# The second layer's unrolled blocks become a counted loop on four engines

## The reference

```python
# attention: q, k, v are (8 batches, 8 heads, 576 positions, 64)
k_p, v_p = means of k, v over groups of 8 positions        # 72 keys per head
attn = softmax(q @ k_p.T / sqrt(64)) @ v_p
x = attn, laid out as (4608 tokens, 512 features)

h = x @ w_in1                                              # 512 -> 2048
g = where(h >= 1, h, where(h <= -1, 0, (h + 1)**2 / 4))
x2 = g @ w_out1                                            # 2048 -> 512

h = x2 @ w_in2                                             # 512 -> 2048
g = h - tanh(h)
y = g @ w_out2                                             # 2048 -> 512
```

## Time and profile before

| | |
|---|---|
| median of 3 runs | 1790.83 us (1788.91 to 1792.78) |
| the profiled execution | 1790.83 us, its span 1788.9 us |
| TensorE busy | 1737.6 us of the span, 97% |
| VectorE, ScalarE busy | 876.1 us, 543.5 us |
| instructions | 24545 |
| granted TensorE clock, mean | 0.994 |

### The profile page before, as it was taken

How to read it: one execution, slowest core, us unless ns; L and a number is a source line. 1 busy time by engine, 2 the same in 40 slices (tenths; PEclk the granted TensorE clock), 3 DMA queues, 4 the chain that set the end, 5 groups by cost and what they waited for, 6 DMA issues and landing times.

```text
span 1788.9 us, 24545 instructions
## 1 busy us (share of the span) xinstructions
PE 1737.6 (97%) x10480; PEld 1575.3 (88%) x10480; DVE 876.1 (49%) x1745; ACT 543.5 (30%) x1141; POOL 160.5 (9%) x136
## 2 busy tenths in 40 slices
PE   4999999999999999999999999999999999999998
PEld 4999999999999999999999888888888888888887
DVE  6585675766856757668544222222222222222222
ACT  3533333333333333333335222222222222222221
POOL 4700011001100110011006100000000000000000
PEclk8999999999999999999999999999999999999999
DMA  5411012001110020111014101010101010101000
GB/s 170 149 60 64 20 34 77 26 26 66 39 64 26 27 77 26 57 34 39 14 65 138 60 0 48 0 48 0 48 0 48 1 47 1 47 1 47 1 24 24
DMA packets 47628, 78.12 MB, mean 44 GB/s; under 512 B 3488, under 2 KB 19872, under 8 KB 47520
## 3 DMA queue, kind: packets, MB, share of 16 engines
q1 hardware_dynamic: 47520, 76.56, 13.2%
HBM read 57.67 MB, written 18.87 MB: 43 GB/s over the span
## 4 chain that ended last, share of the span: by engine, by line
PE 88%; DVE 8%; ACT 2%; DMA 1%; issue 1%; POOL 0%; SPq 0%; DVEq 0%
PE acc_ps L499 42%; PE h_ps L489 30%; PE att_ps L489 6%; PE score_ps L489 6%; PE score_ps L514 2%; DVE v_sum L860 1%; PE score_ps L534 1%; DVE bent L818 1%; DVE g_lo L811 1%; PE att_ps L526 1%; DVE v_tail L882 1%; DVE h_ps L824 1%; DVE prob L896 1%; DVE row_sum L903 1%; DVE row_max L888 1%; ACT prob L698 1%
## 5 line engine op out<-in xcount | busy, mean ns | idle before, releaser
L499 PE MATMUL acc_ps<-g_hi,wout_hi 128*128 128x288 f32 (+1 forms) x1600 | 540.7, 338 | 5.8 <-ACT prob L698 5.8
L499 PE MATMUL acc_ps<-g_hi,wout_lo 128*128 128x288 f32 (+1 forms) x1600 | 529.4, 331 | 0.0
L499 PE MATMUL acc_ps<-g_lo,wout_hi 128*128 128x288 f32 (+1 forms) x1600 | 529.2, 331 | 0.0
L489 PE MATMUL h_ps<-x_hi,win_hi 128*128 128x288 f32 (+1 forms) x1312 | 423.9, 323 | 17.1 <-DVE g_lo L811 12.9
L489 PE MATMUL h_ps<-x_hi,win_lo 128*128 128x288 f32 (+1 forms) x1312 | 416.9, 318 | 0.0
L489 PE MATMUL h_ps<-x_lo,win_hi 128*128 128x288 f32 (+1 forms) x1312 | 414.1, 316 | 0.0
L499 PEld LDWEIGHTS acc_ps<-g_hi,wout_hi 128*128 128x128 f32 x1600 | 302.7, 189 | 34.7 <-ACT prob L698 9.3
L499 PEld LDWEIGHTS acc_ps<-g_lo,wout_hi 128*128 128x128 f32 x1600 | 303.4, 190 | 25.4
L499 PEld LDWEIGHTS acc_ps<-g_hi,wout_lo 128*128 128x128 f32 x1600 | 302.5, 189 | 24.2
L489 PEld LDWEIGHTS h_ps<-x_hi,win_hi 128*128 128x128 f32 x1312 | 247.0, 188 | 35.2 <-DVE g_lo L811 17.4
L489 PEld LDWEIGHTS h_ps<-x_lo,win_hi 128*128 128x128 f32 x1312 | 248.3, 189 | 12.9
(11 more groups left out here) (121 smaller groups left out, 1750.6 us busy)
## 6 DMA issues: line engine op xcount, KB each, us to landing
stage<-kT SPq DMA_DIRECT2D x16, 576.0 KB, 6.0
q_sb<-qT SPq DMA_DIRECT2D x16, 576.0 KB, 4.0
x2T_scratch<-prob SPq DMA_DIRECT2D x16, 576.0 KB, 3.7
x_lo<-x2T_scratch SPq DMA_DIRECT2D x9, 1024.0 KB, 8.4
yT<-out_sb SPq DMA_DIRECT2D x9, 1024.0 KB, 5.1
stage<-v SPq DMA_DIRECT2D x8, 1024.0 KB, 8.6
stage<-w_in SPq DMA_DIRECT2D x8, 1024.0 KB, 5.1
stage<-w_out SPq DMA_DIRECT2D x8, 1024.0 KB, 5.4
```

The source lines that it names most:

```text
L489: last = nc.tensor.matmul(h_bank(j, layer)[:, 0:WIDTH[layer]], w[:, c, j * P:(j + 1) * P], x[:, c, 0:WIDTH[layer]], start=(c == 0 and i == ...
L499: last = nc.tensor.matmul(acc_ps[:, m, 0:WIDTH[layer]], w[:, j, m * P:(m + 1) * P], g[:, j % GRING, 0:WIDTH[layer]], start=(j == 0 and i = ...
```

## The change

On SP, TensorE, ScalarE and VectorE the Python loop over `b`, which wrote the four pairs of blocks out one after the other, becomes `Fori`, a loop that the engine itself runs: the body (two blocks) stands in the program once, a register counts `b`, and a compare-and-branch at the end jumps back while `b` is below 12. Everything computed from `b` (the wait thresholds, the DMA addresses) is computed by the engine from that register. The operations, their order on each engine and their data stay the same. Each of the four engines makes three jumps back, after blocks 17, 19 and 21. The last block and all of layer 1 stay written out.

```diff
@@ sync
-            for b in range(BATCH, BATCH + BLOCKS2 // 2):
+            with sp.Fori(BATCH, BATCH + BLOCKS2 // 2) as b:
                 load_x2_next(2 * b, 0)
                 store_y(2 * b)
                 load_x2_next(2 * b + 1, 1)
                 store_y(2 * b + 1)
@@ tensor
             pe.wait_ge(w_split, 2 * NW - 2)
-            for b in range(BATCH, BATCH + BLOCKS2 // 2):
+            with pe.Fori(BATCH, BATCH + BLOCKS2 // 2) as b:
                 block_body(2 * b, 0, 2)
                 block_body(2 * b + 1, 1, 2)
             block_body(BLOCKS + BLOCKS2 - 1, 0, 2, last=True)
@@ scalar
-            for b in range(BATCH, BATCH + BLOCKS2 // 2):
+            with act.Fori(BATCH, BATCH + BLOCKS2 // 2) as b:
                 block_body(2 * b, 0, 2, x2_next=2 * b + 1 - BLOCKS)
                 block_body(2 * b + 1, 1, 2, x2_next=2 * b + 2 - BLOCKS)
@@ vector
-            for b in range(BATCH, BATCH + BLOCKS2 // 2):
+            with dve.Fori(BATCH, BATCH + BLOCKS2 // 2) as b:
                 block_body(2 * b, 0, 2, x2_next=2 * b + 1 - BLOCKS)
                 block_body(2 * b + 1, 1, 2, x2_next=2 * b + 2 - BLOCKS)
```

## The result

The changed kernel takes 1812.94 us (1811.37 to 1814.03) against 1790.9 us: ratio 1.0124, 95% interval 1.0109 to 1.0139, 22 us slower. The forecast was 1797.4 us in a range of 1789 to 1802: the direction was right, the size more than three times too small. The profiled execution of the changed kernel has a span of 1806.9 us, 18.0 over the span before; the timed ones ran at a mean clock of 0.988 to 0.989 against its 0.991, so they lost more than it shows, and what follows explains the 18.

What follows compares the result with a forecast made beforehand. The prediction took TensorE's matmuls to bound the kernel. Three jumps back, each 3.4 us refill + 0.4 us register work - 1.6 us cover = 2.2 us, add 6.6 us to 1790.8: 1797.4 us, range 1789 to 1802.

Steps and rivals of the forecast that it cites:

- The bound: Second layer: TensorE is busy throughout, so a loop costs time only where it leaves TensorE without an instruction.
- the cover: At TensorE's block end: queued weight loads and matmuls keep the array running 1.6 us after the sum-bank wait.
- Register arithmetic: TensorE's waits: at most 0.2 us a step, hidden, 0 us; next to the jump some 8 operations, 0.4 us.
- the other engines: Jumps of ScalarE, VectorE and SP: refills of 3.4 us at once hidden by 5.2 us slack, SP's too: 0 us.
- the gate chain: ScalarE and VectorE work for the first tile behind the jump: ends 1168.9 us, needed at 1174.12, so 0 us.
- The first refill: TensorE's jump back to code that has gone: 3.4 + 0.4 - 1.6 = 2.2 us idle, 6.6 us for three.
- the sequencer must wait for one packet.: At TensorE's jump, if the target code has gone: one instruction packet is awaited, 3.4 us before the cover is subtracted.
- touch seven or eight: Argument against the no-change rival: the 6.3-packet body touches seven or eight, so a four- or six-packet store would drop its start.
- The clock: Behind TensorE's idle stretches: a lower clock might lose 1.7 us a jump; none in the sum, 5.1 us in the upper bound.
- The range: Whole kernel: 1789 to 1802 us, with 0.1 left above and 0.03 below.
- Both upper bounds together: Whole kernel: 13 us for dearer refills at three jumps plus 5.1 us for the clock, 1809 us.
- no change: the loop's start is still there: Rival at TensorE's jump: memory keeps seven or more packets, 0.4 us hides under 1.6 us of cover, 1790.8 us; chance 0.40.

Runs made afterwards that it cites:

- e1_pe_only: Against the changed kernel, only TensorE keeps its loop; SP, ScalarE and VectorE are written out again: 1812.58 us, ratio 1.0121 to the kernel before.
- four-block loop: Against the changed kernel, TensorE's loop runs over four token blocks, twice, one jump; head at slot 0: 1793.37 us, slot 192: 1793.18 us, slot 228: 1796.28 us.

## Why the prediction was wrong

**The bound and the cover: right.** Only what left TensorE without instructions cost, and the lower clock behind it. The cover of 1.6 us is confirmed twice: at the jump the array ran on for 1.6 us behind the end of the wait (1166.0 + 0.05 to 1167.38 + 0.23), and with the jump moved to where the lead is 3.8 us the stall was gone.

**Register arithmetic, the other engines, the gate chain: right, 0 us.** The register operations take 29 to 63 ns, near the 51 assumed, and the loops on the other engines measured 1.0002. Their jumps missed nothing.

**The first refill: right in kind, a little small.** Forecast 3.4 + 0.4 - 1.6 = 2.2 us of idleness a jump. The branch held the sequencer for 3.9 to 4.4 us (3.39 us away from the transfers); at the first jump the matmuls begin 2.6 us later than they would have (the chain's 2.47 us of issue, plus the modelled 0.39 us of the last matmul less the 0.23 us that it takes). With the other two jumps' idle matmul stretches, 2.25 and 2.73 us, and the same 0.16 on each, that is 7.9 us against 6.6. Taken alone it would have given 1798.7 us.

**The step that failed: "the sequencer must wait for one packet."** It waits for one packet, and 18 instructions on for the next: the head lay at slot 238, and 238 + 1582 = 1820 is over 1792. The prediction had written, as an argument about the rival, that 6.3 packets of body "touch seven or eight", but drew nothing from it for the price: with eight touched and the head near its block's end, the second block is as much gone as the first, and there are eight matmuls to cover what takes 4.5 to 5.4 us. From restart to restart the three jumps took 5.2, 5.4 and 4.5 us for 8 x 0.231 = 1.9 us of work: 3.4 + 3.5 + 2.7 = 9.6 us, where the sum had nothing. This is the largest part of the price.

**The clock: a term left out of the sum.** It was given 1.7 us a jump in the upper bound and none in the sum. The clock fell behind all three jumps. Most of it overlapped with the second stall and cost nothing more there; what remains of the 18.5 us is 18.5 - 7.9 - 9.6 = 1.0 us, about what the first jump explains, where seven matmuls behind the second restart (1175.72 to 1178.67) took 2.95 us instead of 1.62, 1.3 us lost. In the timed executions, 4 us longer at a lower mean clock, it was probably more. The trace of e1_pe_only, the same loop on TensorE in an execution of 1811.65 us at a mean clock of 0.989, shows how: there the lower level lasted 3.4, 3.4 and 10.2 us and fell almost wholly behind the second restarts, where it cost 1.6 + 1.6 + 2.7 = 5.9 us. Its window at the third jump:

```profile
1540.50:1550.70 10.20, 8.38 (x21) 6.31 (x20) 0.00 (x0) 0.00 (x0) 0.00 (x0) 0.50 0.19 72
```

**The range.** Its upper end, 1802, took up one refill and one or two clock stretches. Both upper bounds together were stated as 1809 and even these lie below the median.

**The rival "no change: the loop's start is still there"** was a true account of the memory, and false here only by the place of the head: of the 256 slots at which the loop could have begun, 0 to 210 (1792 - 1582) would by this count keep the body on seven blocks. That the forecast's side, at 0.50 against 0.40, was the right one is luck in this respect: nothing before the change showed the slot. The Trainium skill's two sentences (Runtime: NRT & Kernel Launch, Instruction fetch mechanics) can now be told apart: the 2,048 instructions for TensorE agree with the eight blocks of 256 that the runs show to be kept; the two-page window does not hold for TensorE, where jumps six blocks back met their code in place.

## What to carry to other kernels

A loop on TensorE cost nothing while its body, counted from the start of the block in which its head lies, fitted beside the one block fetched ahead; past that each iteration fetches everything again, so give a long loop the prefetch hint or place its head. Price a jump to code that has gone against the work queued at that point, and put the jump where the sequencer is far ahead, not behind a wait for data. When code may have gone, ask of the block after the target too: a head just before a block's end was the worst place tried.

## What the runs showed of the hardware

- TensorE kept eight blocks of 256 instructions: seven of a loop and the one ahead (slots 0 and 192), or eight of a loop with the hint; at slots 228 and 238, eight and one ahead, the loop was fetched again in full, 92 and 91 packets against 65 and 64.
- A jump back on TensorE to code that was in place took 0.21 to 0.26 us, the entry into a placed loop 0.32 to 0.36, the long loop's jump with the hint 0.38; one to code that had gone, 3.4 to 4.4 us (13 jumps), of which the 16 KB packet itself is a small part (1.7% of 16 engines x 4 us = 1.1 us at the changed kernel's first jump). In a loop on SP, ScalarE or VectorE, 0.04 to 0.07 us.
- The block behind a target that was missed became usable 4.5 to 5.4 us after the restart, at slots 228 and 238 and beside a store and a load of 1 MB; what it takes away from such transfers was not measured.
- The effect is a step: 36 instructions' shift of the same code changed the kernel by 14 us.
- A granted clock of 0.50 for 3.4, 6.8 or 10.2 us followed idle stretches of 2.1 to 2.9 us in several jumps, and not in others with idle stretches as long (slots 192 and 228 of the four-block loop).
